# Cluster similarities with the centroids as stationary operand in four 32-column groups, and the next raw load ahead of the values

## The chip, the cores and the metric

The kernel runs on one core of one Trainium2 chip. The metric is the device time of one execution in microseconds; before the change the median of three runs is 670.88 us (670.83 to 672.24). A core has a matrix engine (TensorE, PE in the profile; its weight loads are listed as PEld), VectorE (DVE), ScalarE (ACT), GpSimd (POOL) and SyncE (SP), which here only issues DMAs. Each takes its instructions in program order and waits on semaphores. TensorE writes to PSUM, eight banks of 128 partitions by 512 float32.

## The reference, cut to what matters

Clustered attention over 2 x 8 heads (768 tokens of 64 numbers), then two mixer blocks over the joined heads. The change touches the part that assigns queries and keys to one of 16 clusters:

```python
q_n = q / (np.linalg.norm(q, axis=-1, keepdims=True) + 1e-06)   # k_n, c_n likewise
q_assign = np.argmax(np.einsum('bhsd,hcd->bhsc', q_n, c_n), axis=-1)
k_assign = np.argmax(np.einsum('bhsd,hcd->bhsc', k_n, c_n), axis=-1)
mask = q_assign[:, :, :, None] == k_assign[:, :, None, :]
scores = scale * np.matmul(q, k.transpose(0, 1, 3, 2))
scores = np.where(mask, scores, -1000000000.0)
scores = scores - np.max(scores, axis=-1, keepdims=True)
attn = np.exp(scores)
attn = attn / (np.sum(attn, axis=-1, keepdims=True) + 1e-09)
return np.matmul(attn, v).astype(np.float32)
...
h = np.maximum(xt @ w_tok1, 0.0) @ w_tok2                        # first mixer, then a channel block
theta = x @ w_theta                                              # second mixer, with cos and sin
```

A positive scale of a query or key doesn't change its argmax, so the kernel takes the similarities from the unnormalised (and scaled) ones.

## The kernel before, in words

The 16 heads are worked on as eight pairs. A pair has 12 steps s: j = s // 6 is the head of the pair, t = s % 6 its tile of 128 queries. Per step TensorE makes the scores of the step after next (`next_score`, four matmuls of 384 columns, L492 and L493), transposes the step's probabilities in two triples (L500), and in the steps with t = 1, 2, 4, 5 multiplies transposed probabilities by values (L508, L509). Two steps per head also transpose the output (L515). ScalarE takes the exponential (L832) and copies the transposed probabilities out as their high part (pt_hi, L801). VectorE takes the row maximum (L1097) and computes the low part (pt_lo, L1133), which frees the PSUM bank for the next triple of transposes. `x_out` on GpSimd scales outputs (L403). The order on each engine is written out by hand; pairs 1 to 6 are a hardware loop, pair 0 and pair 7 stand outside.

While pair p is worked on, pair p + 1 is prepared:

- SyncE: `load_qk` loads raw queries and keys into `raw` (both heads, 128 partitions = 2 x 64 dimensions, 768 tokens), `load_v` the values; `stack` and `oh_in` copy prepared parts from one place of SBUF to another.
- GpSimd: `scale_q` (L364) scales the raw queries, `split_qk` (L354, L386) and `split_v` (L354, L396) split into high and low parts. In pair 0 it also splits two chunks of the weight tok1 and tok2 (L354, L260).
- TensorE: `sims(p + 1, side)`, twice in step 3 (queries before the transposes, keys after): six float32 matmuls each, in which 128 tokens of `raw` are the stationary operand and the pair's two times 16 centroids (32 columns of `cen_t`) move. They write bank 7 with tokens on partitions. A float32 matmul is issued as two instructions, so the trace lists 12 for six (L474).
- VectorE: `argmax` in five pieces (L1079 to L1092) turns bank 7 into one-hot rows; pieces 0, 1, 2 stand in step 3, piece 3 in step 4, piece 4 in step 6.
- TensorE: `oh_transpose` in step 7 (L483, bfloat16); ScalarE: `rows_out` into `oh_rows`.

The first pair's similarities are made before the loop, from `raw0`.

Of the kernel before, what the change touches and what calls it, by code (L numbers as in the profile page):

```python
# [15 lines left out]
F32 = mybir.dt.float32  # L16
# [28 lines left out]
def clustered_mixer(nc, q, k, v, cent, tok1, tok2, ch1, ch2, theta_w, tok_r, tok_i, ch, out):  # L45
    with ExitStack() as ctx:
# [21 lines left out]
        with ExitStack() as a:  # L68
# [3 lines left out]
            with ExitStack() as a1:  # L72
# [8 lines left out]
                onehot = sb(a1, "onehot", [P, NT, 2, 2, 2 * C], BF16)  # L81
# [6 lines left out]
                cen_t = sb(a1, "cen_t", [P, 2, P], F32)  # L88
                cen = sb(a1, "cen", [P, H // 2, C], F32)
# [47 lines left out]
        s_cen_t = sem("s_cen_t")  # L137
        s_sims = sem("s_sims")
# [128 lines left out]
        def _(sp):  # L267
# [21 lines left out]
            def oh_in(p, j):  # L289
                sp.wait_ge(s_oh_rows, p + 1)  # L290
                for dst, side in ((qb, 0), (kb, 1)):
                    r = j * D + side * 2 * C
                    sp.dma_start(dst[D:D + C, j, :].bitcast(F32), oh_rows[r:r + C, :].bitcast(F32)
                                 ).then_inc(s_oh_in[j], 16)
# [11 lines left out]
            def pair(p, last=False):  # L306

                sp.wait_ge(s_score, 12 * p + 6)
                stack(p + 1, 0)
                sp.wait_ge(s_v_split, 2 * p + 2)  # L310
                load_v(p + 1)
                oh_in(p + 1, 0)
                if not last:
                    sp.wait_ge(s_sims, p + 3)
                    load_qk(p + 2)
                sp.wait_ge(s_score, 12 * p + 12)
                stack(p + 1, 1)
                oh_in(p + 1, 1)
# [19 lines left out]
        def _(pool):  # L338
# [68 lines left out]
            def pair(p, first=False, scaled=True, last=False, weights=()):  # L407
# [14 lines left out]
                if scaled:  # L422
                    scale_q(p + 2)
                for n in weights[1:2]:
# [5 lines left out]
            scale_q(1)  # L430
            split_v(0, 0, first=True)
# [25 lines left out]
        def _(pe):  # L457
# [7 lines left out]
            def sims(p, side, src=raw, bank=7, first=False):  # L465

                if side == 0 and not first:
                    pe.wait_ge(s_oh_rows, p)
                    pe.wait_ge(s_cen_t, 4)
                    pe.wait_ge(s_qk_c, p)  # L470
                groups = ps[:, bank, 0:24 * C].rearrange("p (t j s c) -> p t j s c", t=NT, j=2, s=2)
                centroids = cen_t[:].rearrange("p b c -> p (b c)")[:, bass.ds(p * 2 * C, 2 * C)]
                for t in range(NT):
                    mm = pe.matmul(groups[:, t, :, side, :], src[:, side, t * P:(t + 1) * P],  # L474
                                   centroids.rearrange("p (j c) -> p j c", j=2), start=True, stop=True)
                if side == 1 or first:
                    mm.then_inc(s_sims, 1)

            def oh_transpose(bank=7):

                rows = ps[:, bank, 0:HS].bitcast(BF16)
                for t in range(NT):
                    mm = pe.transpose(rows[:, t * P:(t + 1) * P],  # L483
                                      onehot[:, t, :, :, :].rearrange("p j s c -> p (j s c)"), identb[:])
# [69 lines left out]
            def pair(p, first=False, last=False):  # L554
                for s in range(12):
# [10 lines left out]
                    if s == 3 and not last:  # L566
                        sims(p + 1, 0)
# [9 lines left out]
                    if s == 3 and not last:  # L577
                        sims(p + 1, 1)
# [21 lines left out]
            sims(0, 0, src=raw0, first=True)  # L600
            pe.wait_ge(s_raw_k0, 16)
            sims(0, 1, src=raw0, bank=4, first=True)
# [196 lines left out]
        def _(act):  # L799
# [18 lines left out]
            def mask_rows_first():  # L818

                act.wait_ge(s_oh_t, 2)  # L820
                act.activation(kb[D:D + C, 0, :], ps[2 * C:3 * C, 5, 0:HS].bitcast(BF16), ACT.Copy,
# [23 lines left out]
            def pair(p, first=False, last=False):  # L845
                for s in range(12):
# [28 lines left out]
            act.wait_ge(s_oh_zero, 9)  # L875
# [131 lines left out]
        def _(dve):  # L1007
# [4 lines left out]
            for r in range(4):  # L1012
                rows = slice(2 * C * r, 2 * C * r + 2 * C)
                dve.memset(oh_scale[rows, :], BIG if r % 2 else 1.0).then_inc(s_oh_zero, 1)
                dve.memset(oh_bias[rows, :], -BIG if r % 2 else 0.0).then_inc(s_oh_zero, 1)
# [34 lines left out]
            hot = onehot[:].rearrange("p t j s c -> p (t j) s c")  # L1050

            def argmax_first(side):

                r = slice(12 * side, 12 * side + 12)
                sim = ps[:, 4 if side else 7, 0:24 * C].rearrange("p (n s c) -> p n s c", s=2, c=C)[:, :, side, :]
                shape = [P, 12, C]
                dve.wait_ge(s_sims, side + 1)
                dve.tensor_reduce(am1[:, r], sim, AX.X, ALU.max).then_inc(s_am0, 1)
                dve.wait_ge(s_am0, 4 * side + 1)
                dve.tensor_tensor(sim, sim, am1[:, r].unsqueeze(2).broadcast_to(shape),  # L1060
                                  ALU.is_ge).then_inc(s_am0, 1)
                dve.wait_ge(s_am0, 4 * side + 2)
                dve.tensor_tensor(sim, sim, order[:].unsqueeze(1).broadcast_to(shape),
                                  ALU.mult).then_inc(s_am0, 1)
                dve.wait_ge(s_am0, 4 * side + 3)
                dve.tensor_reduce(am2[:, r], sim, AX.X, ALU.max).then_inc(s_am0, 1)
# [3 lines left out]
                dve.tensor_tensor(hot[:, :, side, 0:C], sim, am2[:, r].unsqueeze(2).broadcast_to(shape),  # L1070
                                  ALU.is_equal).then_inc(s_onehot, 1)

            def argmax(p, step):
# [16 lines left out]
                if step == 4:  # L1090
                    dve.wait_ge(s_am, 4 * p)
                    dve.tensor_tensor(hot.rearrange("p n s c -> p (n s) c")[:, :, 0:C], sim, am2[:].unsqueeze(2).broadcast_to(shape),  # L1092
# [25 lines left out]
            def pair(p, first=False, last=False):  # L1118
                for s in range(12):
# [25 lines left out]
                    if not last:  # L1145
                        for step in {3: (0, 1, 2), 4: (3,), 6: (4,)}.get(s, ()):
# [172 lines left out]
```

## Time and profile before

| what | value |
|---|---|
| median of 3 runs | 670.88 us |
| profiled execution | 670.66 us |
| its span | 668.9 us |
| TensorE (matmul) busy | 662.2 us, 99% |
| VectorE busy | 381.4 us, 57% |
| ScalarE busy | 320.8 us, 48% |
| GpSimd busy | 192.0 us, 29% |
| mean granted clock of TensorE | 0.997 |

The span is that of one profiled execution; the 1.8 us around it are in the execution's time and not in the span. A busy share over the whole span mixes stages: the attention (up to about 260 us) keeps VectorE and ScalarE nearly full, the two mixers after it are almost TensorE alone. The chain of waits is followed back from the last instruction; its shares say on whose work the end depends. A matmul's duration in the trace runs until its end is modelled, longer than the distance to the next matmul, since they are pipelined: what an instruction costs the engine is read from the starts. "Idle before" and a releaser in brackets say how long an engine stood still and who ended it.

### The profile page before, as it was taken

How to read it: one execution, taken by the hardware profiler on the slowest of the kernel's cores; microseconds unless marked ns; L12 is line 12 of the kernel's file. 1: busy time of each engine (PE TensorE's matmuls, PEld its weight loads, DVE VectorE, ACT ScalarE, POOL GpSimd, SP SyncE). 2: the span in 40 equal slices, each digit the busy share in tenths (PEclk: the TensorE clock that was granted, in tenths of full speed). 3: DMA queues.
4: the chain of work that ended last, by engine and by line, in shares of the span. 5: the costliest groups of instructions: out<-in, count | busy, mean ns of one | idle time of the engine just before them, and what ended most of it. 6: DMA issues, size and time to landing. Idle time of an engine off the chain costs nothing.

```text
span 668.9 us, 11359 instructions
## 1 busy us (share of the span) xinstructions
PE 662.2 (99%) x4071; PEld 638.4 (95%) x4071; DVE 381.4 (57%) x650; ACT 320.8 (48%) x619; POOL 192.0 (29%) x140
## 2 busy tenths in 40 slices
PE   8999999999999999999999999999999999999998
PEld 8899999999999998999999999999999999999997
DVE  5999898989999885552122122322388246561142
ACT  5787878878787885254102102202677135520010
POOL 5875455362525953025000000200244000060000
PEclk8999999999999999999999999999999999999999
DMA  5586545547464511104000000100431000000022
GB/s 218 103 199 186 132 96 127 151 90 184 82 165 94 129 48 48 48 1 141 17 1 1 1 0 0 47 0 1 142 95 52 12 1 2 0 1 1 1 94 95
DMA packets 16976, 46.92 MB, mean 70 GB/s; under 512 B 3024, under 2 KB 5072, under 8 KB 16944
## 3 DMA queue, kind: packets, MB, share of 16 engines
q1 hardware_dynamic: 16944, 46.48, 26.0%
q8 instruction: 22, 0.36, 0.2%
q14 instruction: 10, 0.08, 0.0%
HBM read 24.15 MB, written 3.15 MB: 41 GB/s over the span
## 4 chain that ended last, share of the span: by engine, by line
PE 98%; DVE 1%; ACT 1%; issue 0%; POOL 0%; POOLq 0%
PE ps L460 20%; PE ps L462 20%; PE ps L461 20%; PE ps L500 10%; PE ps L508 5%; PE ps L509 5%; PE ps L492 5%; PE ps L493 5%; PE ps L474 3%; PE ps L515 2%; PE ps L588 1%; PE ps L728 1%; PE ps L646 1%; PE ps L483 1%; DVE neg_max L1097 0%; DVE pt_lo L1133 0%
## 5 line engine op out<-in xcount | busy, mean ns | idle before, releaser
L801 ACT ACTIVATE pt_hi<-ps 128x384 fp32r<-128x384 f32 x192 | 85.0, 489 | 39.3 <-PE ps L500 38.4
L1133 DVE TENSOR_TENSOR pt_lo<-ps,pt_hi 128x384 fp32r<-128x384 f32 x192 | 97.3, 548 | 7.5 <-ACT pt_hi L801 6.2
L1097 DVE TENSOR_REDUCE neg_max<-ps 128x1 f32<-128x768 f32 x96 | 91.0, 949 | 17.5 <-PE ps L493 16.9
L920 ACT ACTIVATE g_s<-ps 128x384 fp32r<-128x384 f32 x48 | 23.6, 492 | 138.9 <-PE ps L462 138.9
L832 ACT ACTIVATE prob<-ps,neg_max 128x768 f32<-128x768 f32 x96 | 86.8, 904 | 5.7 <-DVE neg_max L1097 5.7
L462 PE MATMUL ps<-u_s,ch_s 128*128 128x384 f32 (+1 forms) x256 | 85.5, 334 | 0.0
L460 PE MATMUL ps<-u_s,ch_s 128*128 128x384 f32 (+1 forms) x256 | 85.5, 334 | 0.0
L461 PE MATMUL ps<-u_s,ch_s 128*128 128x384 f32 (+1 forms) x256 | 85.5, 334 | 0.0
L500 PE MATMUL ps<-ident,prob 128*128 128x128 f32 x576 | 82.3, 277 | 0.6 <-DVE pt_lo L1133 0.5
L500 PEld LDWEIGHTS ps<-ident,prob 128*128 128x128 f32 x576 | 66.6, 142 | 10.1 <-issue 2.4
L1197 DVE TENSOR_TENSOR act_u<-ps,act_u 128x384 f32<-128x384 f32 (+1 forms) x32 | 16.9, 555 | 99.5 <-PE ps L462 99.5
L492 PE MATMUL ps<-ka,qa 128*128 128x384 f32 x192 | 70.5, 367 | 0.6 <-ACT prob L832 0.5
L1192 DVE SCALAR_TENSOR_TENSOR g_s<-ps,g_s 128x384 fp32r<-128x384 f32 x48 | 26.7, 557 | 73.3 <-ACT g_s L920 73.3
L508 PE MATMUL ps<-pt_lo,v_s 128*128 128x384 f32 x192 | 67.7, 353 | 0.1
L493 PE MATMUL ps<-kb,qb 80*128 80x384 f32 x192 | 65.1, 339 | 0.0
L509 PE MATMUL ps<-pt_hi,v_s 128*128 128x384 f32 x192 | 64.8, 337 | 0.0
L462 PE MATMUL ps<-g_s,ch_s 128*128 128x384 f32 x192 | 64.2, 334 | 0.0
L460 PE MATMUL ps<-g_s,ch_s 128*128 128x384 f32 x192 | 64.2, 334 | 0.0
L461 PE MATMUL ps<-g_s,ch_s 128*128 128x384 f32 x192 | 64.2, 334 | 0.0
L460 PEld LDWEIGHTS ps<-u_s,ch_s 128*128 128x128 f32 x256 | 48.1, 188 | 0.0
L461 PEld LDWEIGHTS ps<-u_s,ch_s 128*128 128x128 f32 x256 | 48.1, 188 | 0.0
L462 PEld LDWEIGHTS ps<-u_s,ch_s 128*128 128x128 f32 x256 | 48.1, 188 | 0.0
(147 smaller groups left out, 1377.1 us busy)
## 6 DMA issues: line engine op xcount, KB each, us to landing
stage<-ch_dram SPq DMA_DIRECT2D x9, 768.0 KB, 4.4
qa<-pair_s SPq DMA_DIRECT2D x30, 192.0 KB, 3.1
ka<-pair_s SPq DMA_DIRECT2D x30, 192.0 KB, 4.0
raw<-q_dram SPq DMA_DIRECT2D x8, 384.0 KB, 3.2
raw<-k_dram SPq DMA_DIRECT2D x8, 384.0 KB, 4.3
raw_v<-v_dram SPq DMA_DIRECT2D x8, 384.0 KB, 4.1
out_dram<-act_u SPq DMA_DIRECT2D x16, 192.0 KB, 1.9
qb<-pair_s SPq DMA_DIRECT2D x15, 192.0 KB, 3.4
```

Source lines behind the costliest of these rows:

```text
L460: pe.matmul(o, a_lo, b_hi, start=start, stop=False)
L461: pe.matmul(o, a_hi, b_lo, start=False, stop=False)
L462: return pe.matmul(o, a_hi, b_hi, start=False, stop=stop)
L492: pe.matmul(o, qa[:, j, t * P:(t + 1) * P], ka[:, j, keys], start=True, stop=False)
L493: mm = pe.matmul(o, qb[0:D + C, j, t * P:(t + 1) * P], kb[0:D + C, j, keys], start=False, stop=True)
L500: mm = pe.transpose(ps[:, 4 + u, i * P:(i + 1) * P], prob[:, slot, (HT * u + i) * P:(HT * u + i + 1) * P], ident[:])
L508: pe.matmul(ps[:, 6, 0:HS], va, pt_lo[:, half, t, :], start=(t == 0), stop=False)
L509: mm = pe.matmul(ps[:, 6, 0:HS], va, pt_hi[:, half, t, :], start=False, stop=(t == NT - 1))
L801: return act.activation(o, i, ACT.Copy)
L832: act.activation(prob[:, slot, :].rearrange("p (c k) -> p c k", c=2), ps[:, 2 * slot:2 * slot + 2, 0:HS], ACT.Exp, bias=neg_max[:, s:s + 1 ...
L1097: dve.tensor_reduce(neg_max[:, s:s + 1], ps[:, 2 * slot2:2 * slot2 + 2, 0:HS], AX.XY, ALU.max, negate=True).then_inc(s_max, 1)
L1133: dve.tensor_tensor(pt_lo[at], ps[:, 4 + u, 0:HS].rearrange("p (k q) -> p k q", k=HT), pt_hi[at], ALU.subtract).then_inc(s_pt_lo, 1)
```

## The change

For pairs 1 to 7 the operands of the similarities change places. The 32 centroid columns of the pair, copied by GpSimd into `cen_p` (`centroids_of`, behind `scale_q`), are the stationary operand; 384 tokens of `raw` move. Four float32 matmuls (queries and keys, two halves of the tokens) write bank 7 at partitions 0, 64, 32 and 96, each in its own group of 32 columns of the array. They stand in step 0 of pair p, before its transposes. ScalarE copies the result to `sim_rows` in step 0, and TensorE transposes it in three 128x128 transposes behind the transposes of step 1, which puts tokens on partitions again. VectorE's argmax piece 0 moves from step 3 to step 1. The order of the one-hot columns changes from head, side to side, head, and with it the row numbers in `oh_in`, `mask_rows_first` and the constants `oh_scale`, `oh_bias` (two memsets each instead of four). On SyncE, `load_qk(p + 2)` moves ahead of the wait for the value split, of `load_v` and of `oh_in`. The first pair's similarities keep their form.

TensorE, steps 2 and 3 of a pair in the loop. `qa`, `ka`, `qb`, `kb` are the split queries and keys, `prob` the probabilities, `o_t` the output. Before:

```order
L500 MATMUL ps<-ident,prob 128x128 x6
L515 MATMUL ps<-ident,o_t 128x128 x3
L535 REGISTER_ALU
L492 MATMUL ps<-ka,qa 128x384
L493 MATMUL ps<-kb,qb 128x384
L492 MATMUL ps<-ka,qa 128x384
L493 MATMUL ps<-kb,qb 128x384
L468 REGISTER_ALU
L474 ISA
L474 MATMUL ps<-cen_t,raw 128x2x16 x6
L575 ISA
L500 MATMUL ps<-ident,prob 128x128 x6
```

A second `L474 ... x6` follows there. The similarities stand on both sides of the transposes of step 3; after the change nothing stands there but the scores and the transposes.

TensorE, end of step 0 and step 1 of a pair in the loop, after the change (L528 are the transposes of the probabilities, L536 and L537 the products with the values):

```order
L496 MATMUL ps<-raw,cen_p 32x384 x4
L603 ISA
L528 MATMUL ps<-ident,prob 128x128 x6
L563 REGISTER_ALU
L520 MATMUL ps<-ka,qa 128x384
L521 MATMUL ps<-kb,qb 128x384
L520 MATMUL ps<-ka,qa 128x384
L521 MATMUL ps<-kb,qb 128x384
```

```order
L528 MATMUL ps<-ident,prob 128x128 x6
L504 MATMUL ps<-ident,sim_rows 128x128 x3
L536 MATMUL ps<-pt_lo,v_s 128x384
```

Four wide matmuls now stand ahead of the transposes of step 0, and three transposes of `sim_rows` behind those of step 1.

SyncE, the middle of the loop, between the two `stack`s, before:

```order
L287 DMA kb<-pair_s 64x768
L310 ISA
L278 ISA
L278 DMA raw_v<-v_dram 128x768
L290 REGISTER_ALU
L293 DMA qb<-oh_rows 16x768
L293 DMA kb<-oh_rows 16x768
L314 REGISTER_ALU
L269 ISA
L269 DMA raw<-q_dram 128x768
L270 DMA raw<-k_dram 128x768
```

and after:

```order
L292 DMA kb<-pair_s 64x768
L316 REGISTER_ALU
L274 ISA
L274 DMA raw<-q_dram 128x768
L275 DMA raw<-k_dram 128x768
L318 ISA
L283 ISA
L283 DMA raw_v<-v_dram 128x768
L298 DMA qb<-oh_rows 16x768
L298 DMA kb<-oh_rows 16x768
```

The loads of raw queries and keys moved past the value load and the two small copies. The diff, cut to its core:

```diff
@@ sync: pair
                 sp.wait_ge(s_score, 12 * p + 6)
                 stack(p + 1, 0)
+                if not last:
+                    sp.wait_ge(s_sims, p + 3)
+                    load_qk(p + 2)
                 sp.wait_ge(s_v_split, 2 * p + 2)
                 load_v(p + 1)
                 oh_in(p + 1, 0)
-                if not last:
-                    sp.wait_ge(s_sims, p + 3)
-                    load_qk(p + 2)
@@ gpsimd
+            def centroids_of(p, first=False):
+                if not first:
+                    pool.wait_ge(s_cen_t, 4)
+                    pool.wait_ge(s_sim_pe, p - 1)
+                pool.tensor_tensor(cen_p[:], cen_t[:].rearrange("p b c -> p (b c)")[:, bass.ds(p * 2 * C, 2 * C)],
+                                   one[:].broadcast_to([P, 2 * C]), ALU.mult).then_inc(s_cen_p, 1)
...
                 if scaled:
                     scale_q(p + 2)
+                    centroids_of(p + 2)
@@ tensor
+            def sims(p):
+
+                pe.wait_ge(s_oh_rows, p)
+                pe.wait_ge(s_cen_p, p)
+                pe.wait_ge(s_qk_c, p)
+                for side in range(2):
+                    for half in range(2):
+                        r = (2 * half + side) * 2 * C
+                        mm = pe.matmul(ps[r:r + 2 * C, 7, 0:HS], cen_p[:], raw[:, side, half * HS:(half + 1) * HS],
+                                       start=True, stop=True)
+                mm.then_inc(s_sim_pe, 1)
+
+            def sims_transpose(p):
+
+                pe.wait_ge(s_sim_rows, p)
+                for t in range(HT):
+                    mm = pe.transpose(ps[:, 7, t * P:(t + 1) * P], sim_rows[:, t * P:(t + 1) * P], ident[:])
+                mm.then_inc(s_sims, 1)
...
-                    if s == 3 and not last:
-                        sims(p + 1, 0)
+                    if s == 0 and not last:
+                        sims(p + 1)
...
-                    if s == 3 and not last:
-                        sims(p + 1, 1)
+                    if s == 1 and not last:
+                        sims_transpose(p + 1)
@@ scalar: pair
+                    if s == 0 and not last:
+                        act.wait_ge(s_sim_pe, p + 1)
+                        copy(sim_rows[:], ps[:, 7, 0:HS]).then_inc(s_sim_rows, 1)
@@ vector
-            for r in range(4):
-                rows = slice(2 * C * r, 2 * C * r + 2 * C)
+            for side in range(2):
+                rows = slice(side * D, (side + 1) * D)
...
-                        for step in {3: (0, 1, 2), 4: (3,), 6: (4,)}.get(s, ()):
+                        for step in {1: (0,), 3: (1, 2), 4: (3,), 6: (4,)}.get(s, ()):
                             argmax(p + 1, step)
```

## Rows read from the trace of the kernel before

**Rows 1.** The page: busy time by engine, and the chain that ended last.
```profile
PE 662.2 (99%) x4071; PEld 638.4 (95%) x4071; DVE 381.4 (57%) x650; ACT 320.8 (48%) x619; POOL 192.0 (29%) x140
...
PE 98%; DVE 1%; ACT 1%; issue 0%; POOL 0%; POOLq 0%
```

**Rows 2.** Windows, one loop turn: stretch, length, busy per engine, clock, DMA share, GB/s.
```profile
83.44:113.40 29.96, 29.93 (x214) 28.55 (x213) 27.21 (x50) 23.96 (x54) 13.58 (x14) 1.00 0.53 125
```

**Rows 3.** Chain of waits around step 3: start us, us, engine, output, line.
```profile
83.79 0.33 PE ps L515 x3
...
84.66 0.18 PE ps L493
84.84 1.26 PE ps L474 x12
86.10 0.69 PE ps L500 x6
86.79 1.26 PE ps L474 x12
```

**Rows 4.** Single lines: instructions, duration ns min/median/max, first and last start, forms.
```profile
L493 PE MATMUL ps<-kb,qb x192: 334/338/345, 15.7 to 247.4; 80*128 80x384 f32 x192
...
L483 PE MATMUL ps<-identb,onehot x54: 219/219/314, 10.7 to 217.2; 128*128 128x128 bf16 x54
...
L500 PE MATMUL ps<-ident,prob x576: 270/272/330, 19.5 to 252.4; 128*128 128x128 f32 x192
...
L474 PE MATMUL ps<-cen_t,raw x192: 192/276/401, 6.9 to 207.4; 128*128 x144, 128*128 128x32 f32 x48
```

**Rows 5.** VectorE's timeline, steps 3 to 5: start us, us, instruction, idle before.
```profile
83.17 0.96 DVE L1097 TENSOR_REDUCE neg_max<-ps 128x1 f32<-128x768 f32 x1 [0.53 <-PE ps L493]
...
87.02 1.02 DVE L1133 TENSOR_TENSOR pt_lo<-ps,pt_hi 128x384 fp32r<-128x384 f32 x2 [0.64 <-ACT pt_hi L801]
88.08 0.56 DVE L1079 TENSOR_REDUCE am<-ps 128x24 f32<-128x384 f32 x1
...
89.28 0.57 DVE L1085 TENSOR_TENSOR ps<-ps,order 128x384 f32<-128x384 f32 x1
...
93.20 1.01 DVE L1133 TENSOR_TENSOR pt_lo<-ps,pt_hi 128x384 fp32r<-128x384 f32 x2
```

**Rows 6.** TensorE's timeline: transposes of step 3, second triple of step 6.
```profile
85.94 0.85 PE L500 MATMUL ps<-ident,prob 128*128 128x128 f32 x6
...
94.26 0.31 PEld L500 LDWEIGHTS ps<-ident,prob 128*128 128x128 f32 x3 [0.15 <-DVE pt_lo L1133]
```

**Rows 7.** TensorE's timeline, steps 1 and 2 of pair 0.
```profile
21.38 0.92 PE L500 MATMUL ps<-ident,prob 128*128 128x128 f32 x6 [0.35 <-DVE pt_lo L1133]
...
23.18 0.92 PE L500 MATMUL ps<-ident,prob 128*128 128x128 f32 x6 [0.17 <-DVE pt_lo L1133]
```

**Rows 8.** Timeline, pair 1 into pair 2: SyncE, GpSimd, TensorE.
```profile
62.71 0.71 SPq L278 DMA_DIRECT2D raw_v<-v_dram  x1
...
68.88 0.83 POOL L354 TENSOR_TENSOR v_s<-raw_v,one 128x384 fp32r<-128x384 f32 x1 [1.49 <-PE ps L509]
...
72.09 0.51 POOL L403 TENSOR_TENSOR x_tok<-o_sum,rden 128x192 f32 x1 [1.31 <-DVE o_sum L1103]
...
75.70 1.47 POOL L364 TENSOR_TENSOR raw<-raw,scale 128x768 f32<-128x768 f32 x1 [3.10 <-DMA raw<-k_dram]
...
77.90 1.00 PE L500 MATMUL ps<-ident,prob 128*128 128x128 f32 x6
```

**Rows 9.** Timeline, pair 0 into pair 1: GpSimd, and TensorE's transposes of step 0.
```profile
43.68 3.48 POOL L260 TENSOR_TENSOR tok_s<-stage,tok_s 128x1536 fp32r<-128x1536 f32 x1
...
47.58 1.48 POOL L364 TENSOR_TENSOR raw<-raw,scale 128x768 f32<-128x768 f32 x1
...
47.86 1.00 PE L500 MATMUL ps<-ident,prob 128*128 128x128 f32 x6
```

**Rows 10.** VectorE's timeline before the first pair.
```profile
4.02 0.20 DVE L1024 TENSOR_SCALAR cs<-cs 128x64 f32<-128x64 f32 x1 [1.10 <-ACT cs L804]
```

More of the change, by code:

```diff
@@ L88, in clustered_mixer @@
                 cen_t = sb(a1, "cen_t", [P, 2, P], F32)
+                cen_p = sb(a1, "cen_p", [P, 2 * C], F32)
+                sim_rows = sb(a1, "sim_rows", [P, HS], F32)
                 cen = sb(a1, "cen", [P, H // 2, C], F32)
@@ L137, in clustered_mixer @@
         s_cen_t = sem("s_cen_t")
+        s_cen_p = sem("s_cen_p")
+        s_sim_pe = sem("s_sim_pe")
+        s_sim_rows = sem("s_sim_rows")
         s_sims = sem("s_sims")
@@ L430, in _ @@
             scale_q(1)
+            pool.wait_ge(s_cen_t, 2)
+            centroids_of(1, first=True)
             split_v(0, 0, first=True)
@@ L462, in product, with sims_first @@
                 return pe.matmul(o, a_hi, b_hi, start=False, stop=stop)
[L465 to L472, printed above, removed]
-                for t in range(NT):
[L474 to L477, printed above, removed]
+            def sims_first(side, bank):
+                groups = ps[:, bank, 0:24 * C].rearrange("p (t h s j c) -> p t h s j c", t=HT, s=2, h=2, j=2)
+                for t in range(NT):
+                    mm = pe.matmul(groups[:, t % HT, t // HT, side, :, :], raw0[:, side, t * P:(t + 1) * P],
+                                   cen_t[:, 0, 0:2 * C].rearrange("p (j c) -> p j c", j=2), start=True, stop=True)
+                mm.then_inc(s_sims, 1)
[13 more added lines that the diff above has]
+                    mm = pe.transpose(ps[:, 7, t * P:(t + 1) * P], sim_rows[:, t * P:(t + 1) * P], ident[:])
+                mm.then_inc(s_sims, 1)
             def oh_transpose(bank=7):
@@ L599, in _ @@
             pe.wait_ge(s_q0_scaled, 1)
-            sims(0, 0, src=raw0, first=True)
+            sims_first(0, bank=7)
             pe.wait_ge(s_raw_k0, 16)
-            sims(0, 1, src=raw0, bank=4, first=True)
+            sims_first(1, bank=4)
             for side in range(2):
@@ L820, in mask_rows_first @@
                 act.wait_ge(s_oh_t, 2)
-                act.activation(kb[D:D + C, 0, :], ps[2 * C:3 * C, 5, 0:HS].bitcast(BF16), ACT.Copy,
+                act.activation(kb[D:D + C, 0, :], ps[D:D + C, 5, 0:HS].bitcast(BF16), ACT.Copy,
                                scale=BIG, bias=-BIG).then_inc(s_koh, 1)
@@ L873, in pair @@
                         rows_out(p + 1)
-            act.wait_ge(s_oh_zero, 9)
+            act.wait_ge(s_oh_zero, 5)
             query_rows_first()
@@ L1069, in argmax_first @@
                     dve.wait_ge(s_oh_t, 1)
-                dve.tensor_tensor(hot[:, :, side, 0:C], sim, am2[:, r].unsqueeze(2).broadcast_to(shape),
+                dve.tensor_tensor(hot[:, :, side, :, 0:C], sim, at2.unsqueeze(3).broadcast_to(shape),
                                   ALU.is_equal).then_inc(s_onehot, 1)
@@ L1091, in argmax @@
                     dve.wait_ge(s_am, 4 * p)
-                    dve.tensor_tensor(hot.rearrange("p n s c -> p (n s) c")[:, :, 0:C], sim, am2[:].unsqueeze(2).broadcast_to(shape),
+                    dve.tensor_tensor(hot.rearrange("p t s j c -> p (t s j) c")[:, :, 0:C], sim, am2[:].unsqueeze(2).broadcast_to(shape),
                                       ALU.is_equal).then_inc(s_onehot, 1)
```

26 lines of the change are left out of this document (13 added, 13 removed).

## The prediction

> **What bounds the kernel now.** I read the page first. TensorE (PE) is busy for 99% of the span and makes 98% of the chain of waits [rows 1]; the reader is to see that time is won or lost only by what TensorE issues or waits for. The change lies in the first 250 us, so I went on to a window of one turn of the pair loop, 83.44 to 113.40 us: 29.96 us, TensorE busy 29.93, VectorE (DVE) 27.21, ScalarE (ACT) 23.96, GpSimd (POOL) 13.58, TensorE's granted clock 1.00 [rows 2], that is the 2.4 GHz level. So VectorE is only 2.75 us behind TensorE. Third, the chain of waits around the similarities [rows 3]: 1.26 us for six of them (12 recorded matmuls, as each float32 product is issued as two), six transposes, 1.26 us again, nothing idle between. Then VectorE's timeline after them, TensorE's waits, and the queues of GpSimd and SyncE (SP) at the places where the new order asks for data earlier.
>
> **Removed.** 2 x 1.26 = 2.52 us of TensorE per pair [rows 3], in the seven pairs that prepare a next one: 17.6 us, all on the path. The twelve similarities of the very first pair stay as many and as large.
>
> **Added on TensorE: four products with 384 moving columns.** Each is again two recorded matmuls, so 8 per pair. No row of before has a float32 product that wide, so its price is worked out. A recorded matmul of the same shape in columns, float32r, starts 0.18 us after the one before it [rows 3] and lasts 338 ns; a bfloat16 transpose of 128 columns lasts 219 ns, a float32 one 272 ns, and a float32 similarity of 32 columns that queues behind nothing lasts 192 ns [rows 4]. The 53 ns between the two transposes are 128 more columns at 2.4 GHz, and 192 ns is 219 less 128 columns plus 64: float32 moves each column twice per recorded matmul. For 384 columns that makes 768/2.4 = 320 ns, with the 18 ns that the float32r row has over its 160 ns: 0.338 us each (estimate).
>
> Eight in a row would be 2.70 us. But they go to four different column groups, first and second half of each product to the same group. If groups run independently and matmuls start in program order, the second half of one product waits for its first half, while the first half of the next product can start beside it: 5 slots instead of 8, 5 x 0.338 = 1.69 us. For turning the array from one shape to the other and back I add 0.2 us, between nothing and twice the 0.17 us by which the 338 ns of a matmul exceed its 160 ns of columns. Sum 1.9 us. Bounds: below 5 x 0.178 = 0.9 us (float32 as fast as float32r, no cost of turning), above 8 x 0.338 + 0.34 = 3.0 us (nothing overlaps). The value taken is the middle one since both conditions for the low end contradict rows 4. Seven pairs: +13.3 us.
>
> No matmul of before uses part of the columns, so no row shows overlap or turning. The Trainium skill, TensorEngine Tiling (Array Packing), section Key Properties, says that tiles operate independently but that changing the tiling mode drains the engine; that speaks against the change, and by it the turning would be the full 0.34 us, 1.0 us more in seven pairs. No run here shows it yet.
>
> **Added: three transposes of sim_rows** on TensorE. The same three of o_t take 0.33 us in the chain [rows 3]: 7 x 0.33 = +2.3 us. ScalarE's copy before them (128x384, about 0.5 us) stands between the transposes' copies of step 0 and the next exponential, and TensorE reaches the three transposes a whole step later. ScalarE has 6 us free per pair [rows 2], so I put it at nothing; if the cover failed it would cost at most 0.5 us per pair.
>
> **What is late next: VectorE.** Until now the 2.52 us stood in step 3, just where VectorE has its extra work. In before, VectorE goes from pt_lo of step 3 at 87.02 to the end of pt_lo of step 5 at 94.21, 7.19 us, nearly without a gap: three argmax pieces of 0.56 to 0.57 us, a fourth, two row maxima and three pt_lo [rows 5]. One piece of 0.60 us now moves ahead into step 1, leaving about 6.5. With the 1.08 us from TensorE's transposes of step 3 (85.94) to that pt_lo, the second half of the transposes of step 6 can't start before 7.6 us after those of step 3. TensorE's own work over the same stretch was 94.26 - 85.94 = 8.32 us, with 1.26 of similarities and a wait of 0.15 in it [rows 3, 6]; now 6.9. So a wait of 0.7 us replaces 0.15, and about 0.25 more comes at the transposes of steps 3 and 5, which now follow their pt_lo too closely. I take +0.8 us per pair, 5.6 us in seven. Bounds: 0 (if VectorE gets ahead during steps 0 and 1) and 1.2.
>
> **Pair 0.** Its early steps already wait for pt_lo, 0.35 and 0.17 us [rows 7]; similarities at step 0 cover part of that: -0.3 us.
>
> **Data needed three steps earlier.** sims(p + 1) now needs the scaled queries and cen_p at step 0. In the steady loop GpSimd scaled at 75.70, after 3.10 us of waiting for the load; that load now goes out right behind the stacked copies, where raw_v stood (62.71), so scaling can follow x_out at 72.09 and end near 74.1, cen_p at most 0.5 us later (an x_out, six times as wide, takes 0.51). TensorE gets there at 77.90: 3 us to spare [rows 8]. raw_v goes out about 1 us later behind 0.77 MB; its split waited 1.49 us for TensorE, and x_out behind it another 1.31 us [rows 8], so nothing late reaches the path. In pair 0, though, GpSimd is splitting tok2 until 47.16 and scales from 47.58 to 49.06, while TensorE ends the scores of the next step 0 at 47.86 [rows 9]: one stall of about 1.3 us. Everything queued on TensorE waits with it. The DMA move itself gains nothing but this cover. VectorE's four fewer memsets lie before a wait of 1.10 us for ScalarE [rows 10]: nothing.
>
> **Sum.** -17.6 + 13.3 + 2.3 + 5.6 - 0.3 + 1.3 = +4.6 us. The profiled execution took 670.66 us (span 668.9 and 1.8 around it), 0.2 below the median of 670.88; so 675.5 us.
>
> **Rivals.**
> - *Nothing overlaps.* Float32 halves keep the array to themselves, eight slots: 2.70 + 0.2 = 2.9 us instead of 1.9, +7.0: 682.5 us. For it: in before, every matmul starts 0.17 us or more after the last, none beside another. Against: none of them leaves columns free.
> - *Four at once (not slower).* If halves of all four groups run beside each other, the block costs two slots, 0.68 + 0.2 = 0.9 us: -7.0 against the forecast, 668.5 us. It wins from a block of about 1.2 us down, since 2.52 less 0.33 less 0.8 and a little for pair 0 is what the rest leaves. For it: four different groups. Against: program order and the shared group of each two halves. The Trainium skill, TensorE: Matmul & The Clock Gate, Part 3 (Measured speedup), gives 2.38 times for three column tiles; by that 2.70 would be 1.13 us plus turning and the kernel about 671.5, within reach of no change; no run here has shown it.
> - *VectorE doesn't take over.* It gains a lead in the longer steps 0 and 1 and the 5.6 us don't come: 670 us. Against: its row maximum waits for scores (0.53 us before one at 83.17) [rows 5], so it can't run ahead.
> - *Similarities wait in every pair* for scaled queries or cen_p: each would cost up to the 1.3 us of pair 0, +8: 683 us. Against: 3 us of slack.
>
> **Chances.** Forecast 0.47 (own range 672.5 to 679), nothing overlaps 0.22, four at once 0.15, VectorE doesn't take over 0.11, waiting in every pair 0.05. A measurement of this kernel tells about 0.2% (1.3 us) from no change. Faster by more than that: four at once 0.15 and a part of the third rival, 0.19 in all; within it: the rest of that rival, and the lower tail of the forecast, 0.13; slower 0.68. The range for 8 in 10 goes from the four-at-once time to that of no overlap, 668.5 to 682.5.
>
> **What would show it.** The block of eight matmuls in the chain: 1.7 to 2.1 us (2.7 or more, or about 0.9, is a rival). Starts of its matmuls in pairs a few ns apart or evenly 0.338 us apart. At transposes of steps 5 and 6, TensorE waiting for pt_lo, some 0.7 us, where 0.15 stood. A loop turn of about 30.4 us. One wait for GpSimd at the second pair's step 0. The stages after 260 us keep their length. The forecast is wrong if the turn is under 29.96 us.

## The result, and the profile after

The changed kernel takes 672.7 us (median of 7 runs, 672.17 to 673.67) against 670.83 us before (7 runs on the same chip, 670.07 to 672.24). The ratio is 1.0032, 95% interval 1.0023 to 1.0042: slower by 1.9 us. The forecast was slower by 4.6 us, 675.5 us. The sign and the stated range hold. The size doesn't, and the next table shows that it is the difference of two larger numbers, neither of which was forecast right. The profiled execution took 673.12 us, its span is 671.3 us.

Page of the kernel after: busy time per engine, the granted clock in 40 slices, and the chain that ended last (answers to [rows 1]):

```profile
PE 657.0 (98%) x3980; PEld 621.5 (93%) x3980; DVE 380.4 (57%) x646; ACT 325.3 (48%) x626; POOL 193.3 (29%) x147
...
PEclk9997999999999999999999999999999999999999
...
PE 85%; DVE 5%; issue 4%; ACT 2%; POOL 1%; DMA 1%; SPq 1%; DVEq 0%; ACTq 0%; POOLq 0%
```

TensorE's share of the chain fell from 98% to 85%, and the fourth slice shows a lower clock: there is now time in which the end depends on somebody else. To find it, take one landmark per pair, the start of the first one-hot transpose (L483 before, L511 after), and the distance to the next. From pair 1 on, such a distance is one turn of the loop:

| start of the one-hot transposes in pair | 0 | 1 | 2 | 3 | 4 | 5 | 6 | end of the span |
|---|---|---|---|---|---|---|---|---|
| before, us | 37.23 | 67.17 | 97.26 | 127.16 | 157.08 | 187.00 | 216.91 | 668.9 |
| distance | | 29.94 | 30.09 | 29.90 | 29.92 | 29.92 | 29.91 | 451.99 |
| after, us | 36.68 | 73.59 | 102.76 | 131.93 | 161.12 | 190.31 | 219.48 | 671.3 |
| distance | | **36.91** | 29.17 | 29.17 | 29.19 | 29.19 | 29.17 | 451.82 |

The change wins 0.55 us up to the first landmark and 0.77 us in each of five loop turns, 3.85 us. It loses 6.97 us in one place, between pairs 0 and 1. The rest of the kernel is 0.2 us shorter. Sum: -0.55 + 6.97 - 3.85 - 0.17 = +2.4 us, the difference of the spans of these two executions (the medians differ by 1.9).

**The loop turn.** Windows of the kernel after, one turn; the columns are those of [rows 2]:

```profile
73.59:102.76 29.17, 29.07 (x197) 26.14 (x198) 26.86 (x50) 24.59 (x55) 13.96 (x15) 1.00 0.49 114
```

Chain of waits of the kernel after, the block of step 0 and the transposes of `sim_rows` in step 1 (answers to [rows 3]; start us, us, engine, output, line):

```profile
84.30 0.78 PE ps L496 x8
...
88.32 0.33 PE ps L504 x3
```

And TensorE's timeline of the same place (start us, us, instruction, idle before):

```profile
83.97 0.33 PE L521 MATMUL ps<-kb,qb 80*128 80x384 f32 x1
84.23 0.16 PEld L496 LDWEIGHTS ps<-raw,cen_p 128*32 128x32 f32 x8 [0.25 <-issue]
84.23 0.85 PE L496 MATMUL ps<-raw,cen_p 128*32 128x384 f32 x8
85.01 0.64 PEld L528 LDWEIGHTS ps<-ident,prob 128*128 128x128 f32 x6 [0.62 <-DVE pt_lo L1164]
85.02 0.87 PE L528 MATMUL ps<-ident,prob 128*128 128x128 f32 x6
```

The last score starts at 83.97 and the transposes at 85.02: 1.05 us, of which a score takes 0.18. The block of eight costs 0.87 us of TensorE, where the forecast had 1.9. The two brackets show what happens where the array's shape changes: the weight loads stand still for 0.25 us before the first one of the block, and the transposes' first weight load starts only as the block ends, while elsewhere weight loads run ahead of the matmuls by 0.17 us. (That second wait, 0.62, is put down to pt_lo by the profile; in the experiments below it has the releaser "issue". That both waits come from the change of shape is inferred from their place.)

The merged row hides how the eight matmuls start. TensorE's timeline cut between them shows two groups of four:

```profile
84.23 0.53 PE L496 MATMUL ps<-raw,cen_p 128*32 128x384 f32 x4
...
84.58 0.51 PE L496 MATMUL ps<-raw,cen_p 128*32 128x384 f32 x4
```

A single record is 0.51 us long in the first group and 0.49 in the second, so the four of a group start within some 0.02 us of each other, and the second four 0.35 us after the first. That is neither of the two patterns of the forecast (in pairs, or evenly 0.338 us apart).

Line L496 of the kernel after by itself (answers to [rows 4]; duration in ns, minimum/median/maximum):

```profile
L496 PE MATMUL ps<-raw,cen_p x56: 486/510/848, 17.9 to 201.3; 128*32 128x384 f32 x56
```

Weight loads with TensorE's waits, steps 3, 5 and 6 of pair 2 (answers to [rows 6]):

```profile
92.39 0.31 PEld L528 LDWEIGHTS ps<-ident,prob 128*128 128x128 f32 x3 [0.15 <-DVE pt_lo L1164]
...
97.04 0.31 PEld L528 LDWEIGHTS ps<-ident,prob 128*128 128x128 f32 x3 [0.23 <-DVE pt_lo L1164]
97.51 0.31 PEld L528 LDWEIGHTS ps<-ident,prob 128*128 128x128 f32 x3 [0.15 <-DVE pt_lo L1164]
...
99.30 0.31 PEld L528 LDWEIGHTS ps<-ident,prob 128*128 128x128 f32 x3 [0.38 <-DVE pt_lo L1164]
99.76 0.31 PEld L528 LDWEIGHTS ps<-ident,prob 128*128 128x128 f32 x3 [0.15 <-DVE pt_lo L1164]
```

VectorE's timeline of the kernel after in the same stretch (answers to [rows 5]):

```profile
95.58 0.95 DVE L1128 TENSOR_REDUCE neg_max<-ps 128x1 f32<-128x768 f32 x1
96.44 1.01 DVE L1164 TENSOR_TENSOR pt_lo<-ps,pt_hi 128x384 fp32r<-128x384 f32 x2
97.37 0.54 DVE L1120 TENSOR_REDUCE am<-ps 128x24 f32<-128x384 f32 x1
97.84 0.94 DVE L1128 TENSOR_REDUCE neg_max<-ps 128x1 f32<-128x768 f32 x1
98.70 1.01 DVE L1164 TENSOR_TENSOR pt_lo<-ps,pt_hi 128x384 fp32r<-128x384 f32 x2
```

VectorE has no gap from one row to the next, and TensorE's weight loads wait for it at the steps that the forecast named, with 0.38 and 0.15 us at step 6 where it had 0.7.

**Pair 0 into pair 1.** Timeline of the kernel after: SyncE, GpSimd and TensorE (answers to [rows 9]):

```profile
34.22 0.95 SPq L274 DMA_DIRECT2D raw<-q_dram  x1
35.21 0.95 SPq L275 DMA_DIRECT2D raw<-k_dram  x1
36.20 0.43 SPq L283 DMA_DIRECT2D raw_v<-v_dram  x1
...
42.39 0.83 POOL L359 TENSOR_TENSOR v_s<-raw_v,one 128x384 fp32r<-128x384 f32 x1 [5.54 <-DMA raw_v<-v_dram]
...
42.75 0.41 PE L520 MATMUL ps<-ka,qa 128*128 128x384 f32 x1 [1.17 <-issue]
...
44.26 2.75 POOL L359 TENSOR_TENSOR tok_s<-stage,one 128x1536 fp32r<-128x1536 f32 x1
...
47.08 3.44 POOL L265 TENSOR_TENSOR tok_s<-stage,tok_s 128x1536 fp32r<-128x1536 f32 x1
...
50.94 1.47 POOL L369 TENSOR_TENSOR raw<-raw,scale 128x768 f32<-128x768 f32 x1
52.37 0.24 POOL L376 TENSOR_TENSOR cen_p<-cen_t,one 128x32 f32<-128x32 f32 x1
...
52.71 1.51 PE L496 MATMUL ps<-raw,cen_p 128*32 128x384 f32 x8 [3.83 <-POOL cen_p L376]
```

Read it from the top: raw_v goes out third, GpSimd waits 5.54 us for it, so the split of tok2 ends at 50.52 instead of 47.16, scaling starts 3.4 us later than in [rows 9] and cen_p follows it, and TensorE stands for 3.83 us. Before that it stood for 1.17 us ahead of pair 1's first score. What follows is in the windows of the kernel after (the clock is the number behind GpSimd's group):

```profile
48.00:53.00 5.00, 1.17 (x10) 0.78 (x12) 2.42 (x5) 1.29 (x4) 4.61 (x4) 0.81 0.82 239
53.00:58.00 5.00, 5.00 (x23) 3.86 (x16) 2.25 (x5) 2.24 (x5) 0.75 (x2) 0.51 0.21 88
58.00:73.00 15.00, 14.93 (x99) 13.47 (x99) 13.13 (x25) 11.81 (x26) 8.47 (x7) 1.00 0.51 119
```

TensorE was busy for 1.17 of 5 us, then got a clock of 0.51, about the 1.2 GHz level, for 5 us, and the 2.4 GHz level again after that. Windows of 1 us place it: 1.00 up to 51, 0.54 in the one from 51, 0.50 from 52 to 57, 0.55 in the one from 57, 1.00 from 58. So the clock fell while TensorE still stood. What it cost can be read off: from the start of this block to the next landmark are 20.88 us (52.71 to 73.59), and 18.49 us (50.14 to 68.63) in the first experiment below, where the clock stayed at 1.00. That is 2.4 us; with the two waits, 3.83 and 1.17 us, it makes 7.4.

The trace of the kernel before has a low clock too, elsewhere: 0.83 over 10 to 20 us, where the one after has 1.00. The kernel without the stall, below, has 0.83 there as well and its first landmark at 36.76 us, so this hardly moves the landmarks.

### The profile page after: what moved, and what is told of

It is laid out like the page before. It is cut to its first block, busy times and chain, and to the rows that moved or that the text cites. A ratio compares the mean times of both kernels' runs of the same rounds, so it can differ in the third digit from the quotient of the medians.

```text
span 671.3 us, 11193 instructions
## 1 busy us (share of the span) xinstructions
PE 657.0 (98%) x3980; PEld 621.5 (93%) x3980; DVE 380.4 (57%) x646; ACT 325.3 (48%) x626; POOL 193.3 (29%) x147
## 4 chain that ended last, share of the span: by engine, by line
PE 85%; DVE 5%; issue 4%; ACT 2%; POOL 1%; DMA 1%; SPq 1%; DVEq 0%; ACTq 0%; POOLq 0%
PE ps L477 20%; PE ps L475 20%; PE ps L476 20%; PE ps L528 7%; PE ps L536 4%; PE ps L537 4%; PE ps L520 3%; PE ps L521 3%; DVE pt_lo L1164 2%; DVE neg_max L1128 1%; PE ps L496 1%; PE ps L543 1%; DMA raw_v<-v_dram 1%; ACT pt_hi L829 1%; PE ps L756 1%
## 5 line engine op out<-in xcount | busy, mean ns | idle before, releaser
L528 PE MATMUL ps<-ident,prob 128*128 128x128 f32 x576 | 84.5, 280 | 1.5 <-DVE pt_lo L1164 0.9
L528 PEld LDWEIGHTS ps<-ident,prob 128*128 128x128 f32 x576 | 65.7, 141 | 19.7 <-DVE pt_lo L1164 9.4
L536 PE MATMUL ps<-pt_lo,v_s 128*128 128x384 f32 x192 | 67.9, 354 | 0.1
L537 PE MATMUL ps<-pt_hi,v_s 128*128 128x384 f32 x192 | 65.0, 339 | 0.0
```

Source lines behind the costliest of these rows:

```text
L528: mm = pe.transpose(ps[:, 4 + u, i * P:(i + 1) * P], prob[:, slot, (HT * u + i) * P:(HT * u + i + 1) * P], ident[:])
L536: pe.matmul(ps[:, 6, 0:HS], va, pt_lo[:, half, t, :], start=(t == 0), stop=False)
L537: mm = pe.matmul(ps[:, 6, 0:HS], va, pt_hi[:, half, t, :], start=False, stop=(t == NT - 1))
```

## Experiments

"Before" was run again beside each set of experiments: 670.43 us (18 runs) beside the first four kernels, 670.33 (9 runs) beside the one without the stall, the two on the block and the last one with the moved piece, 670.42 (13 runs) beside the two with the small argmax. The changed kernel's 672.7 us stood beside 670.83. Distances and waits come from one traced execution of each kernel.

### Which part of the stall is the order of the loads

Values first again, everywhere (the edit to SyncE's program of the kernel after):

```diff
                 stack(p + 1, 0)
-                if not last:
-                    sp.wait_ge(s_sims, p + 3)
-                    load_qk(p + 2)
                 sp.wait_ge(s_v_split, 2 * p + 2)
                 load_v(p + 1)
                 oh_in(p + 1, 0)
+                if not last:
+                    sp.wait_ge(s_sims, p + 3)
+                    load_qk(p + 2)
```

> The changed kernel with SyncE's order as before the change (values and one-hot rows ahead of the next raw load), everything else of the change kept. Theory A (the loss sits in pair 0: the value load behind 0.77 MB of raw data delays GpSimd, so the similarities of pair 1's step 0 wait 3.8 us, and the clock falls behind that wait): the stretch from pair 0's to pair 1's one-hot transposes falls from 36.9 to about 31 us, a wait of 1.0 to 1.5 us for cen_p is left, total about 666.7 us, below both kernels. Rival B (the loop needs the early raw load: scaling would end only 0.5 us ahead of the similarities): the five loop turns grow from 29.2 to 30 us or more, total 669 to 671. Rival C (the wide block itself or VectorE is the loss, the order nothing): 672 us, no change.

Measured: 668.38 us, ratio 0.9972 (0.9952 to 0.9992). The distance from pair 0 to 1 is 31.88 us, the turns are 29.2 us. Timeline of this kernel, GpSimd and TensorE:

```profile
39.77 0.83 POOL L359 TENSOR_TENSOR v_s<-raw_v,one 128x384 fp32r<-128x384 f32 x1 [2.85 <-DMA raw_v<-v_dram]
...
50.14 0.85 PE L496 MATMUL ps<-raw,cen_p 128*32 128x384 f32 x8 [2.64 <-POOL cen_p L376]
```

The wait for the values is 2.7 us shorter, the stall 1.2 us, the wait ahead of pair 1's first score is gone, and so is the low clock (1.0 over the span). So the new order of the loads makes 5.0 us of this distance (36.91 less 31.88; nearly all of it is 1.2 of the wait for cen_p, 1.17 of the other and 2.4 of low clock). By the medians it is 3.9 us (1.9 above before and 2.05 below it).

The same with the old order in pair 0 alone (`if first:` around the two places):

> As the first, but SyncE's old order in pair 0 only; in the loop the raw load stays ahead. Theory A: as the first run, about 666.7 us, turns 29.2. If the loop needs the early load (rival B), this one is 3 us or more faster than the first. Rival C: 672 us.

Measured: 669.91 us, ratio 0.9984 (0.9971 to 0.9997), first distance 30.66 us, turns 29.2 us. Both orders give the same turn: at this length of the turn the move is worth nothing in the loop and costs nothing.

The median is not the 666.7 us that was expected, and 1.5 us above the one with the old order everywhere. The ten executions fall into two groups: four with a mean granted clock of 1.000 took 668.18 to 668.69 us, six with 0.992 to 0.997 took 669.89 to 671.37 us. The traced one is of the four (TensorE waited 1.38 us for cen_p; its first landmark came late, at 38.43 us, which is why this wait and the distance are short). The experiment before had one such execution in five, 670.57 us at 0.995. So with the old order in pair 0 a low clock comes in some executions; where in them it lies, no trace shows.

The move alone, put into the kernel before:

```diff
                 stack(p + 1, 0)
+                if not last:
+                    sp.wait_ge(s_sims, p + 3)
+                    load_qk(p + 2)
                 sp.wait_ge(s_v_split, 2 * p + 2)
                 load_v(p + 1)
                 oh_in(p + 1, 0)
-                if not last:
-                    sp.wait_ge(s_sims, p + 3)
-                    load_qk(p + 2)
```

> The kernel before with only SyncE's move. Theory A: GpSimd is about 3.4 us late in pair 0 as well, but the similarities there stand three steps later and don't wait for it; what is left is the wait of about 1.2 us for the one-hot rows queued behind raw data and values: 672 us. Rival (late values alone cost what the changed kernel lost): 675 to 677 us. Rival (the move is neutral or helps): 670.8 or less.

Measured: 672.66 us, ratio 1.0033 (1.0022 to 1.0044); first distance 32.70 us, then 29.9 to 30.2 us. Timeline of this kernel:

```profile
43.52 0.82 POOL L354 TENSOR_TENSOR v_s<-raw_v,one 128x384 fp32r<-128x384 f32 x1 [6.20 <-DMA raw_v<-v_dram]
...
43.91 0.41 PE L492 MATMUL ps<-ka,qa 128*128 128x384 f32 x1 [1.86 <-issue]
```

The same late values, and 1.86 us of TensorE ahead of pair 1's first score, with the old similarities. That score needs the two small copies of one-hot rows, of 48 KB each, which the move puts behind three loads of 384 KB. Their landings show that they are what it waits for. In the kernel after, the second copy (kb, L298) was issued at 38.90 us and landed 3.8 us later, at 42.7; the score started at 42.75. With values first it was issued at 38.97 and landed 2.1 us later, at 41.1; the score started at 41.40 without a wait.

### GpSimd's order in pair 0

In the kernel after, scale_q and centroids_of stand before the split of tok2 in pair 0:

```diff
+                if first:
+                    scale_q(p + 2)
+                    centroids_of(p + 2)
                 for n in weights[0:1]:
                     split_weights(n)
                 x_out(p, 0, 1, 4 * p + 1)
-                if scaled:
+                if scaled and not first:
```

> The changed kernel, SyncE's new order kept; in pair 0 GpSimd scales the next queries and copies the centroids ahead of the split of tok2 (6.2 us). Theory A: cen_p is ready near 46 us, before TensorE asks for it, so wait and low clock go, only the 1.2 us before pair 1's first scores stay: about 667 us. Rival (the wait is for the raw load, not for GpSimd's queue): the wait stays above 2 us, total 670 or more.

Measured: 666.9 us, ratio 0.9944 (0.9928 to 0.9961); first distance 30.62 us; cen_p is ready at 45.91, and TensorE's similarities don't wait for it; 1.13 us ahead of pair 1's first score remain. So the stall of 3.83 us comes from the place of scale_q and centroids_of on GpSimd, behind 6.2 us of splitting.

Both at once: the old order of the loads, and in pair 0 the high half of the tok2 split, then scale_q and centroids_of, then the low half:

> The changed kernel with SyncE's old order (values first) and, in pair 0, GpSimd scaling and copying the centroids between the two halves of the tok2 split. Theory A: neither the wait for cen_p nor the one of 1.2 us before pair 1's scores is left; pair 0 to pair 1 takes about 29.5 us, the other turns 29.2, total 665.7 us. Rival (the raw load lands too late in this order): a wait of 1 us or more stays, 666.7 or more.

Measured: 665.88 us, ratio 0.9932 (0.9918 to 0.9946); all six distances between landmarks are 29.15 to 29.23 us, the span is 663.9 us. Timeline of this kernel (here L504 is the line of the similarities):

```profile
44.36 1.47 POOL L369 TENSOR_TENSOR raw<-raw,scale 128x768 f32<-128x768 f32 x1 [1.19 <-DMA raw<-k_dram]
45.79 0.24 POOL L376 TENSOR_TENSOR cen_p<-cen_t,one 128x32 f32<-128x32 f32 x1
...
47.45 0.85 PE L504 MATMUL ps<-raw,cen_p 128*32 128x384 f32 x8
```

This separates the change into its two halves: without the stall it makes the kernel 5.0 us faster (spans 668.9 and 663.9), and the stall costs 7.4 us (663.9 and 671.3). Those are single traces; by the medians, each beside its own "before", it is 4.5 and 6.3 us.

One thing the move does give in the loop is room. In the kernel after, cen_p is ready 3.4 to 3.6 us before TensorE's block in every loop turn; with the old order, in this kernel, it is 0.4 to 1.1 us.

### What the block of four products costs

All four products in the same 32 columns, so that three of the four results are lost:

```diff
-                        r = (2 * half + side) * 2 * C
+                        r = 0
```

> The changed kernel with all four wide products in the same 32 columns (all write partitions 0 to 31 of bank 7; so three of the four results are lost and partitions 32 to 127 hold old data). Theory A (the 0.87 us block is four groups streaming beside each other, two slots of 320 ns): with one group they follow one another, eight slots of 0.32 to 0.34 us, block 2.6 to 2.9 us, loop turn 29.2 + 1.8 to 2.0 = about 31.1 us, total 672.7 + 12 to 14. Rival (a wide float32 matmul costs 0.1 us wherever it lands, and groups are nothing): block and turn unchanged, 672.7 us.

Measured: 681.64 us (2 runs), ratio 1.0164 (1.0144 to 1.0185); turns 31.04 to 31.14 us. Timeline of this kernel:

```profile
82.48 0.14 PEld L496 LDWEIGHTS ps<-raw,cen_p 128*32 128x32 f32 x2 [0.25 <-issue]
82.48 2.77 PE L496 MATMUL ps<-raw,cen_p 128*32 128x384 f32 x8
82.83 0.11 PEld L496 LDWEIGHTS ps<-raw,cen_p 128*32 128x32 f32 x1 [0.21 <-issue]
83.15 0.11 PEld L496 LDWEIGHTS ps<-raw,cen_p 128*32 128x32 f32 x1 [0.21 <-issue]
...
85.17 0.64 PEld L528 LDWEIGHTS ps<-ident,prob 128*128 128x128 f32 x6 [0.62 <-issue]
```

In one group the weight loads come every 0.32 us, the time that was worked out for 384 columns of float32: eight such slots and about 0.2 us for the change of shape ("turning" in the prediction) are the 2.77 us. In four groups it is 0.85. The turn grew by 1.93 us for a block 1.92 us longer: nothing covers the block. (All four products here also write the same addresses of PSUM; that the slots follow one another for the columns and not for this is argued from their length, 768 cycles of 2.4 GHz.) The total came out lower than expected: the first distance was 34.04 us, not 36.91 plus 1.9. In this trace the values landed 4.6 us after their issue, not 6.1, so cen_p was ready at 51.30 instead of 52.61 us; TensorE came at 49.35 instead of 48.88. It waited 2.05 us instead of 3.83, and its clock stayed at 1.00.

The block issued twice:

```diff
-                for side in range(2):
+                for side in (0, 1, 0, 1):
```

> The changed kernel with the block of four products issued twice, same values, same places. Theory A (two slots per block; 0.87 us = 0.64 + about 0.2 of turning the array, paid once): the block grows by 0.64 to 0.68 us, turn 29.8 us, total +4.5. Rival (the block is limited by how fast eight matmuls start, 48 ns apart): +0.4 us per turn, +2.7. Rival (turning is most of the price): +0.3 or less.

Measured: 677.26 us (2 runs), ratio 1.0099 (1.008 to 1.0118); turns 29.82 to 30.02 us. Timeline of this kernel:

```profile
85.31 0.16 PEld L496 LDWEIGHTS ps<-raw,cen_p 128*32 128x32 f32 x8 [0.26 <-issue]
85.32 1.50 PE L496 MATMUL ps<-raw,cen_p 128*32 128x384 f32 x16
85.66 0.13 PEld L496 LDWEIGHTS ps<-raw,cen_p 128*32 128x32 f32 x4 [0.19 <-issue]
85.99 0.13 PEld L496 LDWEIGHTS ps<-raw,cen_p 128*32 128x32 f32 x4 [0.19 <-issue]
86.74 0.64 PEld L528 LDWEIGHTS ps<-ident,prob 128*128 128x128 f32 x6 [0.62 <-issue]
```

Eight more matmuls cost 0.65 us, two slots of 0.32, and their weights are loaded four at a time, one set per slot. A block is therefore slots of 0.32 us that four matmuls share, plus 0.2 us for the change of shape that doesn't double: 2 x 0.32 + 0.2 is the 0.85 us of the block.

### Is VectorE the bound after the change

Pieces 1 and 2 of the argmax work on one column group of their tile instead of all (the assignments come out wrong), in the kernel without the stall:

```diff
-dve.tensor_tensor(sim, sim, am1[:].unsqueeze(2).broadcast_to(shape), ALU.is_ge).then_inc(s_am, 1)
+dve.tensor_tensor(sim[:, 0:1, :], sim[:, 0:1, :], am1[:, 0:1].unsqueeze(2).broadcast_to([P, 1, C]), ALU.is_ge).then_inc(s_am, 1)
...
-dve.tensor_tensor(sim, sim, order[:].unsqueeze(1).broadcast_to(shape), ALU.mult).then_inc(s_am, 1)
+dve.tensor_tensor(sim[:, 0:1, :], sim[:, 0:1, :], order[:].unsqueeze(1), ALU.mult).then_inc(s_am, 1)
```

> This is the version without the stall of pair 0 (values requested last, the raw work of pair 0 between the two splits of the tokens), with pieces 1 and 2 of the argmax working on one column group of their tile instead of all, so the assignments come out wrong; everything else is as there. Theory (after the change TensorE waits in its steps for VectorE's last piece of P, so VectorE's burst is part of the bound): the waits of TensorE for pt_lo at steps 5 and 6 go, a turn falls from 29.2 to about 28.6 us, and the time is 3 to 4 us under that version (665.9), about 662. Rival (the waits only stand where TensorE would be held anyway): the turn stays at 29.2 and the time at 665.9.

Measured: 661.57 us, ratio 0.9876 (0.986 to 0.9893). Windows of this kernel, one turn:

```profile
93.72:122.26 28.54, 28.51 (x197) 26.26 (x198) 26.20 (x50) 24.44 (x55) 13.78 (x15) 1.00 0.54 132
```

The same cut in the kernel before:

> This is the kernel before with the same two pieces of the argmax on one column group only (the assignments come out wrong), nothing else changed. Theory: before the change TensorE's twelve products of 128 columns at step 3 gave VectorE 2.5 us, so its burst held nothing: the turn stays at 29.9 us and the time within 1 us of 670.4. Rival (VectorE's burst cost the kernel before as much as the one after): the time falls by 3 us or more, to 667.

Measured: 670.32 us, ratio 0.9996 (0.9987 to 1.0006). Windows of this kernel, one turn:

```profile
67.40:97.32 29.92, 29.88 (x211) 28.51 (x211) 26.40 (x50) 23.95 (x54) 13.58 (x14) 1.00 0.53 126
```

The same cut, 0.7 to 0.8 us less of VectorE work, is worth 0.66 us a turn (29.20 to 28.54) after the change and nothing before it. And 28.54 is about what TensorE's own work would leave of the turn of before: 29.92 less 2.52, plus 0.87 and 0.33, is 28.60.

Last, a version that computes everything and only moves a piece: argmax piece 1 from step 3 to step 1, in the kernel without the stall:

```diff
-                        for step in {1: (0,), 3: (1, 2), 4: (3,), 6: (4,)}.get(s, ()):
+                        for step in {1: (0, 1), 3: (2,), 4: (3,), 6: (4,)}.get(s, ()):
```

> As e8, with argmax piece 1 moved from step 3 to step 1 on VectorE. Theory A (after the change VectorE's burst in steps 3 and 4 makes TensorE wait about 0.5 us per turn for pt_lo): piece 1 goes where VectorE has slack, turn 0.3 to 0.4 us shorter than 29.2, total 2 us under e8. Rival (the waits for pt_lo cost nothing): e8's time. Rival (step 1 has no slack either): slower than e8.

Measured: 663.03 us, ratio 0.9891 (0.9876 to 0.9906); turns 28.64 to 28.97 us. Timeline of this kernel, TensorE's weight loads (L504 the similarities, L536 the transposes):

```profile
103.27 0.75 PEld L536 LDWEIGHTS ps<-ident,prob 128*128 128x128 f32 x6
...
105.51 0.19 PEld L504 LDWEIGHTS ps<-raw,cen_p 128*32 128x32 f32 x8 [0.53 <-issue]
```

It is the fastest of those that compute everything, 7.3 us under the kernel before. Its similarities start after 0.53 instead of 0.25 us of idle time in this turn, since TensorE now arrives before cen_p is ready (the turn with this wait is the one of 28.97 us). So with the shorter turn the old order of the loads is at the end of its room.

## Why the prediction was right and wrong

Put side by side, with the terms of the forecast for seven pairs:

| term | forecast, us | measured, us | from |
|---|---|---|---|
| similarities removed | -17.6 | -17.6 | L474 is gone from the loop |
| block of four products | +13.3 | +6.1 | 7 x 0.87, timeline |
| transposes of sim_rows | +2.3 | +2.3 | 0.33 each, chain |
| waits for VectorE | +5.6 | +4.6 (4.4 by medians) | 7 x 0.66, small argmax |
| pair 0, steps 1 and 2 | -0.3 | about 0 | 0.23 and 0.63 us of waits |
| stall at pair 1's step 0 | +1.3 | +7.4 (6.3 by medians) | spans with and without it |
| sum | +4.6 | +2.8 | spans: +2.4 |

- **The block: the step that failed.** The forecast let matmuls start only in program order and made the second half of a product hold back all behind it: "5 slots instead of 8". The price of a slot was nearly right (0.338 us taken, 0.32 measured), and so was the turning, 0.2 us; the count was wrong. Four groups share a slot and the two halves take two, as the rival "four at once" had it with 0.68 + 0.2 = 0.9 us. It had a chance of 0.15, for an argument that no row bore out; the doubled block and the single group settle it. The wrong count is worth -7.2 us; with this term alone put right, the sum would have come out at -2.6 us, on the other side of zero. The Trainium skill (TensorE: Matmul & The Clock Gate, Part 3, Measured speedup) gave 2.38 times for three tiles; here four groups take 0.85 us where one takes 2.77, 3.3 times with the turning included. The page pointed the right way. (The rival "nothing overlaps" also rested on a misreading, that every matmul of before starts 0.17 us or more after the last: in [rows 3] twelve similarities take 1.26 us and six transposes 0.69, so these start 0.11 us apart.)
- **The stall: mechanism right, size far off.** One wait of TensorE for GpSimd at the second pair's step 0 was forecast, with 1.3 us. But it was worked out with GpSimd's times of before, and the late values were dismissed in a sentence on the steady loop ("so nothing late reaches the path"). True in the loop, where both orders give 29.2 us; false in pair 0, where GpSimd has no slack before tok2. The chain that was missed: raw_v third in the queue, issued at 36.20 instead of 34.32 us and landed after 6.1 instead of 4.4; its split late, tok2 late, scale_q late. The cost of 7.4 us splits by the spans of the four combinations: 2.5 us for GpSimd's order alone (666.4 with the old loads, 663.9 without the wait), 1.2 us for the order of the loads alone (665.1), and 3.7 us more when both meet: a late tok2 delays scale_q, and this trace has 2.4 us of low clock. (The split is rough: 665.1 and 663.9 differ also in whether scale_q stands before both halves of the tok2 split or between them.)
- **"The DMA move itself gains nothing but this cover"** was too kind to it: alone it costs 2.2 us (672.66 against 670.43), and in the loop the cover isn't needed while the turn is 29.2 us.
- **VectorE takes over: right.** The places (steps 5 and 6) and nearly the size (0.8 forecast, 0.66 measured) are confirmed by the small argmax, which changes nothing before and takes 0.66 us off a turn after. The rival in which it doesn't take over is refuted, and so is "nothing overlaps" and the wait in every pair: only one of seven blocks waits for cen_p.
- **Duration of a float32 matmul.** The 320 ns of columns worked out from [rows 4] are the distance of the weight loads in one group. The record itself is 486 ns long (510 where it is the first), not 338: in one group too, so the length of a record says nothing on how many run at once.
- **Pair 0.** The forecast let its similarities cover a part of its waits; no such cover shows. A wait of 0.63 us for pt_lo comes at step 3, and the first landmark gains 0.55 us, where 2.52 less 0.87 and 0.33 alone would have given 1.3.

The errors of the two large terms, -7.2 and +6.1 us, nearly cancel. That the sign came out right and the forecast time lies only 2.8 us from the measured one is luck.

## What to carry to other kernels

A move that is free in the steady turn must be priced a second time in the first, unrolled one, where an engine may have another job (here 6.2 us of weight splitting) just ahead of the moved step. Products that leave columns of the array free should be laid side by side, float32 too, and priced by slots, with the change of shape once per block and not once per product. When work of the bounding engine is taken from the step in which a second engine has its burst, the burst has to be spread again in the same change: that one moved piece was worth 2.9 us here.

## What the runs showed of the hardware that was not expected

- Four 32-column groups really run beside each other: 8 float32 matmuls of 384 columns in 0.85 us, 16 in 1.50, against 2.77 for 8 in one group.
- A block of 32-column weights between 128x128 ones costs 0.2 us of TensorE beyond its slots, whether it has two slots, four or eight (0.85, 1.50, 2.77 us): the weight loads stand still for 0.25 us before its first one, and none of the next 128x128 weights is loaded before the block has ended.
- In the stall of 3.83 us, while TensorE stood, the granted clock fell to 0.50 and stayed there until 58 us, 2.4 us lost. The doubled block had a wait of 3.85 us at the same place, and a clock of 0.50 for about 3 us (54 to 57). Waits of 2.64 and 2.05 us there were followed by no such stretch in the executions traced; executions that weren't traced show mean clocks down to 0.992 also where the traced wait was 1.38 us.
- Two copies of 48 KB behind three loads of 384 KB in one queue held TensorE for 1.13 to 1.86 us; in the kernel after, the second of them landed 3.8 us after its issue instead of 2.1.
